# The order in which one queue loads weights, heads and values during the first chunk of an attention plus two-MLP kernel

## The reference

```python
scores = scale * q @ k.T                 # per batch and head
keep   = (pos_k < n_sink) | ((0 <= rel) & (rel < window))
a      = softmax(where(keep, scores, -1e9))
x      = (a @ v)  -> [B*S, H*D] = [1536, 512]
h = x @ w_in;   g = 0 if h <= -1, (h+1)**2/4 between, h if h >= 1;   x = g @ w_out
h = x @ w_in2;  g = h if h > 0 else exp(h) - 1;                      y = g @ w_out2
```

## Time and profile before

| | us |
|---|---|
| median of 3 runs | 655.16 (653.88 to 656.82) |
| the profiled execution, its own time | 653.88 |
| its span, first to last instruction | 652.1 |
| PE matmul busy | 632.1 (97%) |
| DVE busy | 378.1 (58%) |
| ACT busy | 349.8 (54%) |
| PE's share of the chain that ended last | 87% |
| DVE's share of that chain | 9% |

### The profile page before, as it was taken

The page is one execution under the profiler, slowest core; times in us unless marked ns, Lnnn a source line. Parts: engine busy times, 40 slices in busy tenths (PEclk is TensorE's granted clock), DMA queues, the critical chain, the costliest instruction groups (busy, mean ns, idle before and its releaser), DMA issues.

```text
span 652.1 us, 12209 instructions
## 1 busy us (share of the span) xinstructions
PE 632.1 (97%) x4164; PEld 560.2 (86%) x4164; DVE 378.1 (58%) x994; ACT 349.8 (54%) x830; POOL 9.3 (1%) x27
## 2 busy tenths in 40 slices
PE   5789999999999999999999999999999999999997
PEld 3678889999999999999999988888888888888886
DVE  6899968877886788588857863322332222322221
ACT  5777756665765676566656664333443333533333
POOL 3000000000000000000000000000000000000000
PEclk9999999999999999999999999999999999999999
DMA  7765202321331233023044500000100000100001
GB/s 276 229 204 156 72 25 75 93 66 36 90 87 39 63 87 102 25 63 102 0 168 155 194 1 0 1 0 1 65 0 0 0 0 0 64 0 0 0 0 64
DMA packets 24314, 42.47 MB, mean 65 GB/s; under 512 B 2752, under 2 KB 13536, under 8 KB 24288
## 3 DMA queue, kind: packets, MB, share of 16 engines
q1 hardware_dynamic: 24288, 42.13, 20.7%
HBM read 38.98 MB, written 3.15 MB: 65 GB/s over the span
## 4 chain that ended last, share of the span: by engine, by line
PE 87%; DVE 9%; ACT 2%; issue 1%; DMA 0%; ACTq 0%; SPq 0%; DVEq 0%
PE h_ps L516 13%; PE h_ps L514 13%; PE h_ps L515 13%; PE y_ps L529 10%; PE y_ps L531 9%; PE y_ps L530 9%; PE s_ps L531 3%; PE s_ps L530 3%; PE s_ps L529 3%; PE o_ps L497 3%; PE t_ps L477 2%; DVE wout_lo L847 1%; PE s_ps L468 1%; PE s_ps L467 1%; DVE win_lo L847 1%
## 5 line engine op out<-in xcount | busy, mean ns | idle before, releaser
L514 PE MATMUL h_ps<-x_hi,win_hi 128*128 128x256 f32 (+1 forms) x576 | 186.3, 323 | 0.7 <-DVE g_full L873 0.4
L516 PE MATMUL h_ps<-x_hi,win_lo 128*128 128x256 f32 (+1 forms) x576 | 184.8, 321 | 0.0
L515 PE MATMUL h_ps<-x_lo,win_hi 128*128 128x256 f32 (+1 forms) x576 | 183.7, 319 | 0.0
L529 PE MATMUL y_ps<-g_hi,wout_hi 128*128 128x256 f32 (+1 forms) x480 | 147.0, 306 | 1.6 <-DVE g_lo L860 1.6
L531 PE MATMUL y_ps<-g_hi,wout_lo 128*128 128x256 f32 (+1 forms) x480 | 146.4, 305 | 0.0
L530 PE MATMUL y_ps<-g_lo,wout_hi 128*128 128x256 f32 (+1 forms) x480 | 145.9, 304 | 0.0
L877 DVE SCALAR_TENSOR_TENSOR g_full<-g_full,h_ps 128x512 f32<-128x512 f32 x48 | 33.0, 687 | 156.7 <-ACT g_full L682 156.6
L514 PEld LDWEIGHTS h_ps<-x_hi,win_hi 128*128 128x128 f32 x576 | 108.2, 188 | 10.7 <-DVE g_full L873 1.0
L515 PEld LDWEIGHTS h_ps<-x_lo,win_hi 128*128 128x128 f32 x576 | 108.6, 189 | 9.4
L516 PEld LDWEIGHTS h_ps<-x_hi,win_lo 128*128 128x128 f32 x576 | 108.4, 188 | 8.3
L669 ACT CAST g_hi<-g_full 128x256 fp32r<-128x256 f32 (+1 forms) x144 | 68.6, 476 | 68.6 <-DVE g_full L877 34.1
(11 more groups left out here) (105 smaller groups left out, 734.4 us busy)
## 6 DMA issues: line engine op xcount, KB each, us to landing
ks<-in_k SPq DMA_DIRECT2D x40, 260.0 KB, 2.7
raw<-in_w_in SPq DMA_DIRECT2D x11, 512.0 KB, 4.5
raw<-in_w_out SPq DMA_DIRECT2D x11, 512.0 KB, 4.3
qs<-in_q SPq DMA_DIRECT2D x40, 128.0 KB, 2.6
vals<-in_v SPq DMA_DIRECT2D x20, 192.0 KB
out_y<-xy SPq DMA_DIRECT2D x12, 256.0 KB, 2.1
xy<-in_w_in SPq DMA_DIRECT2D x5, 512.0 KB, 7.3
xy<-in_w_out SPq DMA_DIRECT2D x5, 512.0 KB, 4.9
```

Source lines behind the costliest of these rows:

```text
L514: pe.matmul(o, win_hi[:, k, f], x_hi[:, k, :], start=(k == 0), stop=False)
L515: pe.matmul(o, win_hi[:, k, f], x_lo[:, k, :], start=False, stop=False)
L516: last = pe.matmul(o, win_lo[:, k, f], x_hi[:, k, :], start=False, stop=(k == KT - 1))
L529: pe.matmul(o, wout_hi[:, t, cols], g_hi[:, t % GR, :], start=begin, stop=False, skip_group_check=True)
```

## The change

In the SP list the loads for chunk 1 and the weight blocks 5 to 15 are put in another order. No load is added or left out, and no wait is rewritten; each keeps the condition that it had. The other engines' lists are the same. `load_pair(1, p)` is `load_head(1, 2p)`, `load_head(1, 2p+1)`, `load_values(1, p)`.

```diff
             load_head(1, 0)
             load_head(1, 1)
+            load_values(1, 0)
             load_weights(5)
-            load_values(1, 0)
+            load_weights(6)
+            load_head(1, 2)
+            load_weights(7)
+            load_weights(8)
+            load_head(1, 3)
             load_values(1, 1)
-            load_weights(6)
-            load_weights(7)
-            load_head(1, 2)
-
-            load_weights(8)
             load_weights(9)
-            load_weights(10)
-            load_weights(11)
-            load_head(1, 3)
-            load_weights(12)
-            load_weights(13)
-            load_head(1, 4)
-            load_weights(14)
-            load_head(1, 5)
-            load_weights(15)
-            load_values(1, 2)
-            load_head(1, 6)
-            load_head(1, 7)
-            load_values(1, 3)
+            for i in range(10, NW):
+                load_weights(i)
+            load_pair(1, 2)
+            load_pair(1, 3)
             with sp.Fori(2, NC) as c:
```

## The result

The changed kernel takes 657.25 us (median of 12 runs, 656.72 to 661.8), the kernel before 655.18 us on the same chip (12 runs, 653.88 to 657.45). The ratio is 1.0051 with a 95% interval of 1.0033 to 1.0068: 3.3 us slower by the ratio, 2.1 us by the medians, where the forecast was 2.6. The record of this result lists 38 runs of the changed kernel. The median of the 12 lies in the quickest group; that of the 38 is 658.92, 3.7 us above the kernel before.

A forecast was written before the change was run, and what follows sets the result against it. DVE was taken to bound chunk 0 to 82 us, PE after it. Costs 0 (front) + 2.6 (head 4) + 0 (rest) on 653.88 gave 656.5, or 657.8 us by the median 655.16; range 655.0 to 660.4.

The forecast's parts named there:

- The bound: Chunk 0, about 26 to 82 us: DVE has no slack, so any stop delays PE's start at 82.36 equally.
- The sign that nothing would differ before 53 us: In the changed profile, the three compute engines would look as before up to 53 us.
- What has room: Front of the new load list, blocks 5 to 15, values and head 3: loads land in time, cost 0.
- Head 4: Step 8: queries issued behind block 15 land at 57.5, DVE starts at 58.47 instead of 55.88, cost 2.6 us.
- The clock: Rival: behind PE's 3.2 us wait the clock halves for one step, adding 2.5 us, giving 660.3; chance 0.06.
- The base: Starting time the cost was added to: 653.88 us for the profiled execution, the quickest of three, or their median, 655.16.

The follow-up runs named there:

- the smaller dose: The kernel before, with head 4's loads held until the tenth split and issued in front of block 15: 656.47 us, ratio 1.002.
- both fills: The changed kernel with unused PE transposes in the first attention and 24 unused matmuls before head 4's scores: 657.92 us, ratio 1.004.

## Why the prediction was right, and where not

**The bound.** Right. DVE alone sets the pace from 26 to 82 us, and a stop of it reaches the end whole: 1.05 us late gave 1.1 us of span in the smaller dose, and 3.0 late gave 3.0 with both fills. The chain passes to PE 1.1, 3.0, 4.8 and 7.8 us later in the profiles of the smaller dose, of both fills and of the changed kernel's two, and these are the differences of their spans too. The sign that nothing would differ before 53 us did not come true, by the early fall of the clock.

**What has room.** Right: the front of the list at 0 (head 4 put back: ratio 1.0005), no wait for block 5 or for blocks 9 to 11 in any profile.

**Head 4.** Right in mechanism and size. The landing was forecast 4.0 us after the queries' issue; 4.4 and 3.8 us were measured in the changed kernel's two profiles, and 4.1 with both fills. From ACT's start to DVE's start I took 0.97 us; 61.38 to 62.34 is 0.96. The delay was forecast at 2.6 and came out at 3.05 and 2.5 in the two profiles of the changed kernel. By its quickest group the changed kernel is 2.9 us slower (spans from 654.9 against 652.0).

**The clock.** The step that failed is the rival's weight. I gave it 0.06 and named a clock below 1.00 behind the wait as a sign of being wrong. That sign came: the clock did fall in both profiles of the changed kernel, within PE's wait of 3.63 and 3.10 us, and its 18 quickest runs have a mean clock of 0.995 to 0.997, where the quickest of before have 0.999 or 1.000 in nearly all. Its price was wrong the other way. I took one whole step at half clock, less PE's slack, as 2.5 us. A fall of 3.4 us cost 0.1, since PE's slack against DVE took it up, one like it with head 4 alone moved cost 0.3, and one of 6.8 us cost 1.3. The evidence that I set against it, PE's wait of 3.34 us at the start with 1.00 behind it, was no evidence: see the last section. The Trainium skill's sentence that an idle array falls to 1.2 GHz (TensorE: Matmul & The Clock Gate, "What's actually happening") is borne out here by both profiles. The early fall is another case: PE was not idle ahead of it but lightly busy, 0.93 of 2 us from 18 to 20 us.

**The base.** What I called scatter of the runs, 653.88 to 656.82, is two groups, and the sum on the profiled execution stood in the lower one. That the median before, 655.16, lies between the groups is why 657.8 came near the median of 657.25 while the difference by ratio is 3.3 us. This nearness is in part luck: the median of all 38 runs, 658.92, is 1.1 us from the forecast, and the sum had no term for the second fall of the clock.

## What to carry to other kernels

In a queue that works in order, a load's time is set by the slowest wait in front of it: set each load's place by when the wait ahead ends and how long before that its user wants it, and move the one that is late, not the list. Where an engine has no idle time over a stretch, every microsecond of a new wait is a microsecond of the kernel, and the engine that waits behind it may pay again through its clock. Before a difference of half a per cent is explained from one profile, look at the clock of all runs: here the kernel before had two groups 2.5 us apart, as much as the change.

## What the runs showed of the hardware

The record of the granted clock says 1.00 from the start in most profiles, but the first matmuls run at about half speed. The same three groups of PE's work, first in the kernel before, then in the changed kernel's first profile:

```profile
11.70 1.12 PE L434 MATMUL y_ps<-xy 64*128 64x128 f32 x8
12.75 0.87 PE L457 MATMUL o_ps<-probs_t,vals 128*64 128x256 f32 x8
13.55 0.88 PE L444 MATMUL h_ps<-ident,xy 128*128 128x128 f32 x6
```

```profile
11.90 1.65 PE L425 MATMUL y_ps<-xy 64*128 64x128 f32 x8
13.48 1.50 PE L448 MATMUL o_ps<-probs_t,vals 128*64 128x256 f32 x8
14.91 0.87 PE L435 MATMUL h_ps<-ident,xy 128*128 128x128 f32 x6
```

The step to full speed comes later here: the eight value products take 1.50 us and not 0.87. That makes up most of the 1.2 us by which SP's issue at 21.70 is late against 20.47, with the clock at 1.00 in the windows to 20 us. It also fits the group of spans at 653.0 to 653.5 with a mean clock of 1.000 in several of the kernels, which no profile caught. In the changed kernel's second profile the eight products of this kind at 8.85 us take 0.93 us and not 1.65, so PE was at full speed there, and the record shows it fall to 0.50 at 10.2 us. So the record may leave out the slow start and still show every later fall.

POOL's subtraction of 128x1024 floats holds up some of DVE's instructions until it ends: one of 0.69 us took 2.15 us beside it and one of 0.17 us took 1.06, while one that read an input from PSUM kept its 0.42. The Trainium skill (GPSIMD Engine Reference, "8. Key points") names contention on the shared SBUF interfaces for DVE instructions with two SBUF inputs, which `k_lo` is; the trace agrees.
